# Chunked linear attention feeding two expert layers, on one core: the two finest levels and the diagonal leave TensorE, and q and k are turned in 32x32 blocks by VectorE

## The reference

```python
# q, k, v, f_logit: (4, 8, 768, 48)
f = sigmoid(f_logit)
for t in range(S):
    state = f[:, :, t, :, None] * state + einsum('bhd,bhe->bhde', k[:, :, t], v[:, :, t])
    y[:, :, t] = einsum('bhd,bhde->bhe', q[:, :, t], state)
x = y.transpose(0, 2, 1, 3).reshape(3072, 384)
h = x @ w_in                                  # 384 -> 2048
x2 = (h * sigmoid(1.702 * h)) @ w_out         # 2048 -> 384
p = domain_probs / domain_probs.sum(-1)
out = sum over e of p[:, e] * (relu(x2 @ w1[e]) @ w2[e])   # 4 experts, 384 -> 1024 -> 384
```

## Time and profile before

| | us |
|---|---|
| median of 3 runs (1504.25 to 1509.03) | 1507.51 |
| the profiled execution, its own time | 1505.92 |
| its span in the profile | 1504.1 |
| TensorE busy | 1478.5 (98%) |
| VectorE busy | 643.9 (43%) |
| ScalarE busy | 440.9 (29%) |
| GpSimd busy | 434.9 (29%) |

### The profile page before, as it was taken

How to read it: one execution, slowest core, us unless ns; L and a number is a source line. 1 busy time by engine, 2 the same in 40 slices (tenths; PEclk the granted TensorE clock), 3 DMA queues, 4 the chain that set the end, 5 groups by cost and what they waited for, 6 DMA issues and landing times.

```text
span 1504.1 us, 23994 instructions
## 1 busy us (share of the span) xinstructions
PE 1478.5 (98%) x8740; PEld 1397.5 (93%) x8740; DVE 643.9 (43%) x953; ACT 440.9 (29%) x779; POOL 434.9 (29%) x395
## 2 busy tenths in 40 slices
PE   7899999999999999999999999999999999999999
PEld 6899999999999999999999999999999999999998
DVE  8683646556373646523442323332332333233323
ACT  6453434343343434333321211111111112111111
POOL 7684645445453645434200010010001000100000
PEclk9999999999999999999999999999999999999999
DMA  8422222220302221021211000010010100100011
GB/s 150 98 65 45 37 32 49 32 49 10 63 8 42 39 33 32 1 80 35 90 39 42 0 12 31 0 42 0 0 42 0 41 1 0 42 0 0 21 42 63
DMA packets 148624, 52.90 MB, mean 35 GB/s; under 512 B 127056, under 2 KB 143952, under 8 KB 148560
## 3 DMA queue, kind: packets, MB, share of 16 engines
q1 hardware_dynamic: 148560, 51.97, 15.8%
HBM read 42.52 MB, written 9.44 MB: 35 GB/s over the span
## 4 chain that ended last, share of the span: by engine, by line
PE 90%; POOL 3%; issue 3%; DVE 2%; ACT 1%; DMA 0%; SPq 0%; POOLq 0%; DVEq 0%; ACTq 0%
PE bank L1032 12%; PE bank L1031 12%; PE bank L1030 12%; PE bank L1226 9%; PE bank L1224 9%; PE bank L1225 9%; PE bank L1084 8%; PE bank L1171 4%; PE bank L1172 4%; PE bank L1173 4%; PE bank L1118 3%; POOL decays L517 1%; PE bank L1115 1%; PE bank L1128 1%; POOL k_T L558 1%
## 5 line engine op out<-in xcount | busy, mean ns | idle before, releaser
L787 ACT ACTIVATE h_h<-bank 128x512 fp32r<-128x512 f32 x192 | 114.8, 598 | 637.5 <-PE bank L1032 637.5
L1226 PE MATMUL bank<-we_h,h_l 128*128 128x384 f32 x768 | 257.2, 335 | 0.0
L1224 PE MATMUL bank<-we_h,h_h 128*128 128x384 f32 x768 | 257.0, 335 | 0.0
L1225 PE MATMUL bank<-we_l,h_h 128*128 128x384 f32 x768 | 256.9, 334 | 0.0
L984 DVE SCALAR_TENSOR_TENSOR h_l<-bank,h_h 128x512 fp32r<-128x512 f32 x192 | 132.7, 691 | 283.9 <-ACT h_h L787 283.9
L610 POOL TENSOR_TENSOR we_l<-we_raw,we_h (+1 forms) x48 | 63.1, 1315 | 621.7 <-ACT we_h L777 621.7
L592 POOL TENSOR_TENSOR g_l<-sig,g_h 128x384 fp32r<-128x384 f32 x128 | 160.1, 1251 | 268.3 <-ACT g_h L726 268.3
L1032 PE MATMUL bank<-x,we_l 128*128 (+1 forms) x576 | 225.1, 391 | 0.0
L1031 PE MATMUL bank<-x,we_h 128*128 (+1 forms) x576 | 224.9, 391 | 0.0
L1030 PE MATMUL bank<-x,we_h 128*128 (+1 forms) x576 | 224.0, 389 | 0.0
L995 DVE SCALAR_TENSOR_TENSOR acc<-bank,p_n,acc 128x384 f32 (+1 forms) x192 | 105.2, 610 | 266.4 <-PE bank L1226 266.4
(11 more groups left out here) (93 smaller groups left out, 2090.3 us busy)
## 6 DMA issues: line engine op xcount, KB each, us to landing
we_raw<-in_moe_w SPq DMA_DIRECT2D x16, 768.0 KB, 6.1
q_raw<-in_q SPq DMA_DIRECT2D x24, 192.0 KB, 4.0
k_raw<-in_k SPq DMA_DIRECT2D x24, 192.0 KB, 5.0
v_sb<-in_v SPq DMA_DIRECT2D x24, 192.0 KB, 4.4
x_dram<-work SPq DMA_DIRECT2D x8, 576.0 KB, 3.4
x_raw<-x_dram SPq DMA_DIRECT2D x12, 384.0 KB, 4.0
out_dram<-acc SPq DMA_DIRECT2D x5, 768.0 KB, 3.5
f_raw<-in_f_logit SPq DMA_DIRECT2D x56, 48.0 KB, 2.2
```

The lines of the kernel that those rows point to most:

```text
L1224: pe.matmul(dst, hh, wh, start=j == 0, stop=False)
L1225: pe.matmul(dst, hh, wl, start=False, stop=False)
L1226: last = pe.matmul(dst, hl, wh, start=False, stop=j == GT - 1)
```

## The change

The turns of q and k: halves 1 to 7 load them as the gates are loaded, in 16 DMAs each (`load_blocks`), and VectorE turns them with two more `STREAM_TRANSPOSE`, all three ahead of the first `gelu_product` of the half. Half 0 keeps TensorE's turns. The tokens' own products: q, k and f are loaded once more, four tokens (a quad) to a partition (`load_quads`, 24 DMAs), once the raw tiles are free; GpSimd multiplies all pairs within a quad elementwise, VectorE sums them (9 `TENSOR_REDUCE`) into `small`, 16 DMAs from SBUF to SBUF (`load_bands`) spread `small` into `band`, and three predicated copies of 128x1024 per half put `band` into `scores_T`. Levels 0 and 1 keep their fades of `q_T` and `k_T`, but not their `q_split`, matmuls and copies. `v_diag` goes. The weight pieces of half 0 are split after its chunk steps and no longer beside its levels.

```diff
-    plan[0] = [("transpose", "gate"), ("transpose", "q")]
-    plan[1] = [("transpose", "k")]
-    for L in range(LEVELS):
-        plan[3 + L].append(("level", L))
-    for c in range(CH):
-        plan[8 + c] += [("diagonal", c)]
-    plan[10] += [("k_rows", 0)]
+    plan[0] = [("transpose", "gate"), ("transpose", "q"), ("transpose", "k"), ("fade", 0)]
+    plan[1] = [("level", 0)]
+    plan[2] = [("level", 1)]
+    for L in range(FIRST, LEVELS):
+        plan[4 + L - FIRST].append(("level", L))
+    plan[5] += [("quad", "gate"), ("quad", "diagonal")]
+    plan[6] += [("quad", "odd")]
+    plan[7] += [("quad", "cross")]
+    plan[9] += [("k_rows", 0)]
+    plan[10] += [("band", c) for c in range(CH)]
...
+            def load_blocks(b, a, n):
+                sp.wait_ge(small_ready, n * 3 * CH)
+                for dst, src, loaded in ((f_blocks, f_blocks_v, f_blocks_loaded), (q_blocks, q_blocks_v, q_blocks_loaded),
+                                         (k_blocks, k_blocks_v, k_blocks_loaded)):
+                    for r in range(PAIRS):
+                        for i in range(QUADRANTS):
+                            lo = SQ * (i % 2)
+                            width = min(SQ, D - lo)
+                            sp.dma_start(dst[i * SQ:(i + 1) * SQ, r, :, 0:width],
+                                         src[b, a, 2 * r + i // 2, :, :, lo:lo + width]).then_inc(loaded, 16)
...
+            def load_bands(n):
+                sp.wait_ge(small_ready, (n + 1) * 3 * CH)
                 for r in range(PAIRS):
+                    for i in range(QUAD):
+                        sp.dma_start(band[i:P:QUAD, :, 2 * r:2 * r + 2, :],
+                                     small[r * SQ:(r + 1) * SQ, :, i, :, :]).then_inc(bands_loaded, 16)
...
+            load_quads(0, 0, 0)
...
-            load_f(0, 1, 1)
-            for i in range(STAGES, STAGES + IN_ALONE):
-                load_piece(i)
-            load_qk(0, 1, 1)
-            for i in range(STAGES + IN_ALONE, STAGES + ALONE_PIECES):
+            load_bands(0)
+            load_blocks(0, 1, 1)
+            for i in range(STAGES, STAGES + ALONE_PIECES):
                 load_piece(i)
             load_v(0, 1, 1)
+            load_quads(0, 1, 1)
...
+            def load_half(n, b, a, next_b):
+                load_v(b, a, n)
+                store_x2(n - 2)
+                load_quads(b, a, n)
+                load_bands(n)
+                if next_b is not None:
+                    load_blocks(next_b, 1 - a, n + 1)
...
+                if s == "transpose" and c == "q" and not fine(n):
+                    dve.wait_ge(q_blocks_loaded, n * 16 * BLOCK_LOADS)
+                    dve.wait_ge(unit_ready, n * UNITS)
+                    dve.transpose(q_T[:, :].rearrange("p (r t x) -> p r t x", r=PAIRS, x=SQ), q_blocks)\
+                        .then_inc(q_ready, CH)
...
+                if s == "band":
+                    if c == 0:
+                        dve.wait_ge(bands_loaded, (n + 1) * 16 * BAND_LOADS)
...
             def both(n, b, a, n1):
-                step("transpose", "gate", n1, a, b)
+                for t in ("gate", "q", "k"):
+                    step("transpose", t, n1, a, b)
...
+                    pe.wait_ge(band_ready, n * CH + c + 1)
                     if c == 0:
                         pe.wait_ge(qf_ready, (n + 1) * (LEVELS + 1) * CH)
```

More of the change, by code:

```diff
@@ L69, in moe_of_attention_kernel @@
     IN_ALONE, OUT_ALONE = len(win_pieces) // 2, CH
+    after_step = {(s, c): engine for c in range(CH) for s, engine in (("k_rows", "pool"), ("y", "dve"), ("update", "pool"))}
     ALONE_PIECES = IN_ALONE + OUT_ALONE
@@ L249, in moe_of_attention_kernel @@
         plan[12 + 2 * c] += [("update", c)] + [("k_rows", c + 1)] * (c + 1 < CH) + [("x", c)]
[L251 to L253 removed]
+    all_steps = [s for slot in plan for s in slot]
     with ExitStack() as ctx:
@@ L301, in weights_beside @@
                 emit_step(*s, 0, 0, 0)
-                if s[0] == "level" and done < IN_ALONE or s[0] == "update":
+                if s in after_step:
                     emit_piece(done)
@@ L537, in step @@
                     L = c
-                    if L == 0:
-                        pool.wait_ge(read_by["dve"], n * PER_HALF["dve"] + CH)
-                    else:
+                    if L == 0 and not fine(n):
+                        pool.wait_ge(k_ready, (n + 1) * CH)
+                    if L:
                         pool.wait_ge(kg_ready, (n * LEVELS + L) * CH)
@@ new lines, in step @@
+                if s == "quad" and c == "cross":
+                    pool.wait_ge(quad_faded, n * 3 + 3)
+                    for ch in range(CH):
+                        pool.wait_ge(small_ready, n * 3 * CH + CH + ch + 1)
+                        for j in range(2):
+                            last = pool.tensor_tensor(
+                                prod[ch].rearrange("p (s j t d) -> p s j t d", s=2, j=2, t=2)[:, :, j, :, :],
+                                q_quad[:, ch, j, 2:4, :].unsqueeze(1).broadcast_to([P, 2, 2, D]),
+                                k_quad[:, ch, j, 0:2, :].unsqueeze(2).broadcast_to([P, 2, 2, D]), ALU.mult)
+                        last.then_inc(quad_product, 1)
@@ new lines, in step @@
+                if s == "transpose" and c == "k" and not fine(n):
+                    dve.wait_ge(k_blocks_loaded, n * 16 * BLOCK_LOADS)
+                    dve.transpose(k_T[:, :].rearrange("p (r t x) -> p r t x", r=PAIRS, x=SQ), k_blocks)\
+                        .then_inc(k_ready, CH)
+                if s == "transpose" and c == "k" and fine(n):
+                    for ch in range(CH):
+                        dve.wait_ge(gate_ready, ch + 1)
+                        dve.wait_ge(q_ready, ch + 1)
+                        part, by = (t[:, :].rearrange("p (r c m) -> p r c m", r=PAIRS, c=CH)[:, :, ch, :]
+                                    for t in (q_T, gate_T))
+                        dve.tensor_tensor(part, part, by, ALU.mult).then_inc(qf_ready, 1)
@@ new lines, in step @@
+                if s == "fade" and not fine(n):
+                    dve.wait_ge(gate_ready, (n + 1) * CH)
+                    dve.wait_ge(q_ready, (n + 1) * CH)
+                    dve.tensor_tensor(q_T[:, :], q_T[:, :], gate_T[:, :], ALU.mult).then_inc(qf_ready, CH)
+                if s == "quad" and c != "gate":
+                    done = n * 3 * CH + ["diagonal", "odd", "cross"].index(c) * CH
+                    for ch in range(CH):
+                        if c == "diagonal":
+                            dst = small_spots(ch, 0, 1)
+                            src = prod[ch].rearrange("p (j k d) -> p j k d", j=2, k=QUAD)
+                        if c == "odd":
+                            dst = small_spots(ch, 1, 2)
+                            src = prod[ch][:, 0:CHUNK_COLS // 2].rearrange("p (j k d) -> p j k d", j=2, k=2)
+                        if c == "cross":
+                            dst = small[:, ch, 0:2, :, 2:4].rearrange("p s j t -> p (s j) t")
+                            src = prod[ch].rearrange("p (i t d) -> p i t d", i=4, t=2)
+                        dve.wait_ge(quad_product, done + ch + 1)
+                        dve.tensor_reduce(dst, src, AX.X, ALU.add).then_inc(small_ready, 1)
@@ L946, in both @@
                     for s in plan[slot]:
-                        if s != ("transpose", "gate"):
+                        if s[0] != "transpose":
                             step(*s, n1, a, b)
```

289 lines of the change are left out of this document (157 added, 132 removed).

## The result

The changed kernel takes 1578.24 us (median of 4 runs, 1576.44 to 1579.99); the kernel before, beside it, 1506.83 (median of 4). The ratio is 1.0475, 95% interval 1.0451 to 1.0498: slower by 4.7%. The profiled execution has a span of 1578.1 us against 1504.1.

What follows compares the result with a forecast made beforehand. TensorE was taken to bound the turns, latency through VectorE half 0. Half 0 +23, clock +1, turn 1 -2 and turns 2 to 7 -19 made +3 on the profiled 1505.9: median 1510.5 us, range 1488 to 1529.

Steps and rivals of the forecast that it cites:

- What bounds the kernel: Whole kernel: TensorE, busy 98% of the span, bounds the turns; latency through VectorE bounds half 0.
- The sum: Whole kernel: 23 + 1 - 2 - 19 = +3 us on the profiled 1505.9, giving 1510.5 us.
- What TensorE gives up: Each turn: two turns of q and k and two levels leave TensorE, 8.0 us.
- The start of a turn: First slots: TensorE waits 2.0, 1.4 and 1.1 us for product and `g_l`, leaving a turn's gain at 4.4 us.
- The middle of a turn: Slots 5 to 7 and the bands before `y`: costs of 0.3 and 0.9 us per turn.
- GpSimd's crowd: Slots 5 to 7: quad products beside `g_l` and `k_T` on GpSimd cost 0.3 us per turn.
- The bands: Before `y` of chunk 0: 16 DMAs and first band copy make it wait 0 to 2.0 us, taken as 0.9.
- Half 0: Before turn 1: quads, bands, block loads, then weight pieces delay turn 1 to 83.0 us; +23, between +19 and +29.
- Turn 1: Turn with nineteen weight pieces: gain 4.5, less 0.9 for bands and 1.6 for slots 5 to 7; -2 us.
- The second: Rival: quad or band DMAs cost SP 0.57 us or more, delaying half 0 and each turn; 1526 us, chance 0.32.
- Slower: Whole kernel: outcome slower than before, chance 0.42, against faster 0.31 and same 0.27.
- That half 0 and the turns about cancel: Whole kernel, the main forecast: half 0's loss and the turns' gain nearly balance, 1500 to 1518 us, chance 0.38.

Runs made afterwards that it cites:

- kernel 8: The changed kernel with band DMAs issued half by SP, half by ScalarE, and half 0's last two weight pieces ahead of the q and k blocks: 1533.4 us.
- (6): The changed kernel without GpSimd's quad products, VectorE summing the loaded q, k and gates instead (wrong numbers): 1513.4 us.
- (2): The changed kernel with 8 of the 16 band DMAs issued by ScalarE instead of SP: 1536.6 us.
- (12): The changed kernel with pieces ahead (1572.3 us), each quad step one slot earlier and the three 384-element products on VectorE instead of GpSimd: 1544.4 us.
- experiment 5: The changed kernel with 36 extra, unused TensorE transposes of the identity before each turn's wait for the bands of chunk 0: 1560.7 us.
- Experiment 4: The changed kernel with half 0's last two weight pieces loaded ahead of the q and k blocks instead of behind all 48 block loads: 1572.3 us.

## Why the prediction was wrong

**What bounds the kernel** held: TensorE bounds the turns, SP's order half 0's end.

**Where the miss lies.** The sum was +3 us, the profile shows +74. Of the 71 between them turns 2 to 7 hold 55 (a turn gained 3.2 in the forecast and lost 5.9), turn 1 14, half 0 3.

**What TensorE gives up**, 8.0 us a turn, agrees with the trace of before by the starts of the rows: a turn of q moves what follows by 1.3 us, a level by 2.7. But the busy time fell by 6.3 only (77.64 against 83.89, both at full clock). Each wait has a price beside its length: the matmul ahead of it ends 0.16 us behind the next one's usual start (0.33 long, one every 0.17), and the first behind it takes 0.44 instead of 0.33. For the seven waits more of kernel 8's turn 2 that is, as an estimate, 7 x 0.27 = 1.9 us.

**The start of a turn** was right in its size, and nearly in its parts: waits of 1.5, 1.2 and 1.1 us in turn 3 (1.5, 2.2 and 0.4 in turn 2) where 2.0, 1.4 and 1.1 were forecast, and transposes of 1.73 to 1.78 that leave the first of the decays at 1.47. But what `g_l` of slot 0 waited for was the end of the decays, 0.99 us long behind them in turn 3, and not VectorE's fade, which had ended 0.3 us before. By the Trainium skill (SBUF — State Buffer, Who interferes with whom) a VectorE instruction with one SBUF input, outside the 2-port modes, does not contend with GpSimd, and the 1.47 agrees.

**The middle of a turn** is the step that failed, in each of its three terms.
- GpSimd's crowd, 0.3 us: the waits for `k_T` (1.4) and `k_rows` (1.2) came to 2.6, and without the products both are gone (6). The working's own rows said it: 1.70 + 1.57 + 3.8 is 7.1 us of GpSimd in slot 5, and 6.5 and 5.9 in slots 6 and 7, where a slot lasts 5.83. It took each slot by itself, and what is left over in one is carried to the next. And the products took 12.5 us instead of 9.6: 1.0 us for 384 elements, and not the 829 ns of `v_diag`.
- The bands, 0.9 us and 2.0 at most: 4.3 (3.5 in turns 3 and 5). The last sum was forecast 41.4 us behind the turn's start and came at 45.5. The 16 DMAs took 11.0 us and not 5.3 to 9.1: 0.65 us or more each, outside the rows taken as bounds. `y` was wanted 3.9 us later than thought, which hid part of it. Each for itself, the DMAs on two queues (2) and the sum 5 us sooner (12) bring the wait under 0.6 us.
- Nothing at all was put down in turns 2 to 7 for the clock behind that wait, though the earlier trace rows showed what a pause does: 2.7 us a turn by experiment 5.

Together 2.3 + 3.4 + 2.7 = 8.4 us; with 1.7 for what TensorE gave up less and 0.5 less at the start 9.6, where a turn's mean of 90.7 is 9.1 over the 81.6 forecast.

**Half 0**: turn 1 at 83.0 (80 to 88) forecast, 87.1 measured, by the chain that was named. The last sum came at 45.9 (41.2), the bands took 10.5 (7.2), the 48 block loads 25.7 (28.5), the rest 5.0 (6.1). So the total was near because terms missed in both directions, +8.0 and -3.9; that is part luck. The range of +19 to +29 doesn't follow from its own bounds either, whose low ends give +18 and high ends +33. Experiment 4 shows the price of the pieces' place in that order, 7.6 us by turn 2's start.

**Turn 1**, forecast 2 us shorter, was 11.7 longer: waits of 4.4 for `k_T`, 5.1 at its start and 2.1 before `y`, and a clock of 0.89. The weight pieces in the crowded slots were priced at 1.6. What of the low clock belongs to which wait was not tried.

**The rivals.** The second (small DMAs are slow) named the right place and direction, 2 us of band wait a turn and turn 1 at 88, but its 1526 left out the clock in the turns and the crowd. "Slower" had the largest chance of the three, 0.42, by smaller losses than those that came. That half 0 and the turns about cancel was wrong because no turn gained anything: even the best full version (8) has turns of 85.4 us against 84.8, with half 0 and turn 1 still 24 us longer.

No version with all of the computation beat the kernel before. What would take away the start's 4 us stays open.

## What to carry to other kernels

When work moves off the bounding engine into a chain of small steps (products, sums, DMAs, a copy), add the chain up from its first step to its reader, with the load that the helping engine carries from one slot to the next, before counting the gain. Many small DMAs on one queue are a serial cost of their own: price them by a row of their own shape, and split them over two idle queues if they stand on the path. Add up an engine's work in each stretch, and carry over what does not fit. Price a wait of TensorE with the clock behind it: here some 4 us of waiting cost 6.7.
